# Two third-stage matmuls of a transform chunk placed side by side, each with its own accumulator bank

## The reference

```python
X = np.fft.rfft(x, axis=1)
Y = X * (filt_r + 1j * filt_i)[None]
x = np.fft.irfft(Y, n=3008, axis=1).reshape(6016, 256)
rms = np.sqrt(np.mean(x * x, axis=-1, keepdims=True) + 1e-06)
xn = x / rms * rms_g
g, val = xn @ w_gate, xn @ w_val                   # 256 x 1536 each
x = (g / (1 + np.exp(-g)) * val) @ w_out           # 1536 x 256
r = np.maximum(x @ w_in2, 0.0)                     # 256 x 2048
out = (s * (r * r) + b) @ w_out2                   # 2048 x 256
```

## Time and profile before

| | |
|---|---|
| median of 3 runs | 1290.36 us (1289.22 to 1291.53) |
| profiled execution | 1293.23 us, of which the recorded span is 1291.4 us |
| TensorE busy in the span | 1254.6 us (97%) |
| VectorE busy | 685.8 us (53%) |
| ScalarE busy | 564.6 us (44%) |
| GpSimd busy | 165.7 us (13%) |
| mean granted TensorE clock | 0.981 of full speed |

### The profile page before, as it was taken

One profiled execution on the slowest core, in us unless ns is written; L12 is line 12 of the kernel. 1 busy time (PEld: TensorE's weight loads), 2 busy tenths in 40 slices (PEclk: granted clock), 3 DMA queues, 4 the chain that ended last, 5 costly groups with the idle time before them and its releaser, 6 DMA issues.

```text
span 1291.4 us, 20490 instructions
## 1 busy us (share of the span) xinstructions
PE 1254.6 (97%) x7268; PEld 1220.7 (95%) x7268; DVE 685.8 (53%) x1161; ACT 564.6 (44%) x1122; POOL 165.7 (13%) x167
## 2 busy tenths in 40 slices
PE   8976899999999999999999999999999999999998
PEld 5644899999999999999999999999999999999998
DVE  3647345545445544445554366555655555555555
ACT  4625333433333334333344355455554555555544
POOL 5636111110111110111101030000000000000000
PEclk7978899999999999999999999999999999999999
DMA  8470600000000000000001000000000000000000
GB/s 234 136 202 11 177 14 13 13 13 2 10 12 12 12 12 0 12 12 12 0 14 51 1 1 13 13 13 13 12 12 12 12 12 12 12 12 12 4 9 24
DMA packets 20583, 37.91 MB, mean 29 GB/s; under 512 B 2240, under 2 KB 16192, under 8 KB 20288
## 3 DMA queue, kind: packets, MB, share of 16 engines
q1 hardware_dynamic: 20544, 37.40, 10.2%
HBM read 24.94 MB, written 12.45 MB: 29 GB/s over the span
## 4 chain that ended last, share of the span: by engine, by line
PE 89%; POOL 4%; issue 3%; DMA 2%; DVE 1%; ACT 1%; SPq 0%; POOLq 0%; ACTq 0%
PE bank L378 29%; PE bank L379 29%; PE bank L380 29%; POOL spec L877 2%; PE bank L365 2%; DMA by_j<-w_b 1%; POOL f L870 1%; DMA z_ring<-by_j 1%; POOL gate_lo L882 1%; PE bank L344 1%; DMA f<-filt 0%; PE bank L333 0%; PE bank L354 0%; PE bank L374 0%; PE bank L375 0%
## 5 line engine op out<-in xcount | busy, mean ns | idle before, releaser
L755 DVE TENSOR_TENSOR h<-bank,act 128x376 f32<-128x376 f32 x192 | 104.5, 545 | 307.4 <-PE bank L380 299.6
L793 DVE SCALAR_TENSOR_TENSOR h<-act,sc 128x376 f32<-128x376 f32 x256 | 159.5, 623 | 188.5 <-ACT act L621 184.5
L571 ACT ACTIVATE act<-bank 128x376 f32<-128x376 f32 x192 | 93.1, 485 | 374.6 <-PE bank L380 374.5
L621 ACT ACTIVATE act<-bank 128x376 f32<-128x376 f32 x256 | 124.1, 485 | 223.7 <-PE bank L380 223.6
L379 PE MATMUL bank<-h_lo,out_hi 128*128 128x376 f32 x512 | 171.4, 335 | 0.0
L380 PE MATMUL bank<-h_hi,out_lo 128*128 128x376 f32 x512 | 171.3, 335 | 0.0
L378 PE MATMUL bank<-xn_hi,in_hi 128*128 128x376 f32 x512 | 171.1, 334 | 0.2 <-issue 0.2
L378 PE MATMUL bank<-h_hi,out_hi 128*128 128x376 f32 x512 | 171.2, 334 | 0.0
L379 PE MATMUL bank<-xn_lo,in_hi 128*128 128x376 f32 x512 | 171.0, 334 | 0.0
L380 PE MATMUL bank<-xn_hi,in_lo 128*128 128x376 f32 x512 | 170.3, 333 | 0.0
L799 DVE SCALAR_TENSOR_TENSOR h_lo<-h,bi,h_hi 128x376 fp32r<-128x376 f32 x256 | 157.7, 616 | 0.2 <-ACT h_hi L630 0.2
(11 more groups left out here) (79 smaller groups left out, 2078.6 us busy)
## 6 DMA issues: line engine op xcount, KB each, us to landing
x_ring<-x SPq DMA_DIRECT2D x16, 384.0 KB, 5.6
by_j<-w_b SPq DMA_DIRECT2D x4, 1536.0 KB, 13.0
z_ring<-by_j SPq DMA_DIRECT2D x32, 192.0 KB, 2.9
out<-staged SPq DMA_DIRECT2D x32, 188.0 KB, 1.9
f<-filt SPq DMA_DIRECT2D x8, 384.0 KB, 7.8
in_raw<-w_in SPq DMA_DIRECT2D x1, 2048.0 KB, 7.9
out_raw<-w_out SPq DMA_DIRECT2D x1, 2048.0 KB, 8.3
gate_raw<-w_gate SPq DMA_DIRECT2D x1, 1536.0 KB, 13.0
```

Source lines behind the costliest of these rows:

```text
L571: nc.scalar.activation(act[:, c % 2], bank[2 * (c % 2)][:, 0:TILE], ACT.Silu).then_inc(silu_done, 1)
L621: nc.scalar.activation(act[:, c % 2], bank[c % 4][:, 0:TILE], ACT.Relu).then_inc(relu_done, 1)
L755: nc.vector.tensor_tensor(h[:, c % 2], bank[2 * (c % 2) + 1][:, 0:TILE], act[:, c % 2], ALU.mult).then_inc(hmul_done, 1)
L793: nc.vector.scalar_tensor_tensor(out=h[:, c % 2], in0=act[:, c % 2], scalar=sc2[:], in1=act[:, c % 2], op0=ALU.mult, op1=ALU.mult).then_in ...
```

## The change

Both third-stage matmuls of chunk q-1 are issued directly after `step2(q)`, and the first stage of chunk q+1 follows them. The half dp = 1 gets bank 7 in place of bank 6. ScalarE's two `w_out_copy` stand side by side in the same way, ahead of the two `u_out`. Since bank 7 is now shared, waits are added wherever the fourth stage, the sum of squares and the third stage follow each other in it, and `step4(1, 1, 1)` stands behind the last wait for `w_done` in place of ahead of it.

```diff
             def step3(q, dp):
                 pe.wait_ge(spec_done, 2 * q + dp + 1)
-                if q or dp:
-                    pe.wait_ge(w_done, 2 * q + dp)
-                nc.tensor.matmul(bank[6][:, 0:COLS], tabs[:, TB3:TB4], spec[:, q % 2, dp],
+                if q:
+                    pe.wait_ge(w_done, 2 * q + dp - 1)
+                if q in (11, 12, 15) and dp:
+                    pe.wait_ge(y_done, {11: 1, 12: 2, 15: 3}[q])
+                if q == 14 and dp:
+                    pe.wait_ge(var_done, 1)
+                nc.tensor.matmul(bank[6 + dp][:, 0:COLS], tabs[:, TB3:TB4], spec[:, q % 2, dp],
                                  start=True, stop=True).then_inc(s3_mm, 1)
...
                 if q == 12:
                     pe.wait_ge(consts_in, 64)
+                    pe.wait_ge(w_done, 2 * 11)
                     step4(0, 0, 0)
                 if q:
                     step3(q - 1, 0)
+                    step3(q - 1, 1)
                 if q + 1 < ALL:
                     step1(q + 1, 0)
                     step1(q + 1, 1)
-                if q:
-                    step3(q - 1, 1)
                 if q == 12:
+                    pe.wait_ge(w_done, 2 * 12)
                     step4(0, 0, 1)
                 if q == 14:
+                    pe.wait_ge(w_done, 2 * 14)
                     sums(0)
-            pe.wait_ge(var_done, 1)
+            pe.wait_ge(w_done, 2 * 15)
             step4(1, 1, 0)
             gate_val(0, 0, 0)
             step3(ALL - 1, 0)
             gate_val(0, 0, 1)
             step3(ALL - 1, 1)
+            pe.wait_ge(w_done, 2 * ALL)
             step4(1, 1, 1)
-            pe.wait_ge(w_done, 2 * ALL)
...
-                               bank[6][:, 0:COLS].rearrange("p (i g j) -> p j g i", i=PAIRS, g=HALVES)).then_inc(w_done, 1)
+                               bank[6 + dp][:, 0:COLS].rearrange("p (i g j) -> p j g i", i=PAIRS, g=HALVES)).then_inc(w_done, 1)
...
                 if q:
                     w_out_copy(q - 1, 0)
+                    w_out_copy(q - 1, 1)
                 if q + 1 < ALL:
                     u_out(q + 1, 0)
                     u_out(q + 1, 1)
-                if q:
-                    w_out_copy(q - 1, 1)
```

## The result

The changed kernel takes 1293.77 us (median of 16 runs, 1290.81 to 1299.17), the kernel before, run beside it, 1290.43 us (16 runs, 1288.98 to 1294.33). The ratio is 1.0028, 95% interval 1.0018 to 1.0039: slower by 3.3 us. A second measurement of the same pair gave 1.0026 (1.0012 to 1.0040). The forecast was 1292.0 us within 1288.6 to 1295.2, so the time is inside the range, but the likeliest case, no change by 0.2%, did not come. The loss is about twice the 1.66 us of the sum.

What follows compares the result with a forecast made beforehand. TensorE bounds the kernel after 126 us; before that, waits tied to stores and the normalised tile decide. Delays and gains up to `w_out_copy(15, 1)` sum to +1.66 on 1290.36, giving 1292.0 us, range 1288.6 to 1295.2.

Steps and rivals of the forecast that it cites:

- opening, up to turn 2: Before turn 2: one uncovered ScalarE copy starts that turn 0.75 us later, at 25.74.
- six turns from turn 2 to 8: Turns of 5.49 us with the copy uncovered: 32.94 us in place of 30.09; turn 8 starts 3.60 us later overall.
- release of the store within turn 8: The copy releasing batch 0's store comes 3.12 us into turn 8 in place of 4.87, 1.75 earlier.
- store to input of chunk 12: Chunk 12's input still lands 20.38 us behind the start of batch 0's store, SyncE's queue being the same.
- input to turn 12: After the input wait, at the lower clock, no third stage is left: 4.31 us in place of 4.99.
- turn 12: The added wait for `y_done` holds the second third-stage matmul: 8.80 us to turn 13 in place of 7.50.
- turn 15 to the gate product: With its own bank, `w_out_copy(14, 1)` comes 3.12 us into turn 15 in place of 3.98: 0.86 us won.
- I take zero: Nothing added for slow clock returns; upper bounds were 1.8 us after the second restart and 1.0 in turn 12.
- The clock stays up in the shortened wait: Rival, chance 0.10: clock holds through turn 11's halved input wait, taking 3.2 us off, to 1288.8 us.
- The clock falls inside the loop: Rival, chance 0.07: idle of about 0.6 us a turn drops the clock, 4.4 us per turn, 1305 us.
- Late clock: Rival, chance 0.18: clock returns late in turn 12 and after the second restart, adding 2.8 us, 1294.8 us.
- The copy not uncovered: Rival, chance 0.05: only 0.3 us of ScalarE's copy is uncovered, turns take 5.04 us, end 1288.9 us.

Runs made afterwards that it cites:

- the run from turn 8 on: Changed kernel's second bank and waits, old order in turns 1 to 7, new order in turns 8 to 15: 1290.29 us, ratio 0.9998 against the kernel before.
- the run with turn 8 and the clock held: Both banks, new order in turn 8 only, eight extra matmuls ahead of turn 11's first stage: 1286.49 us, ratio 0.9967 against the kernel before.
- the run that held it: Changed kernel plus six extra, never-read matmuls at the end of turn 11: 1289.86 us, ratio 0.9992 against the kernel before.
- `A`: Turn order of the kernel before (third, first, third stage), with the changed kernel's bank and waits; in every turn: 1291.23 us, ratio 1.0006 against before.
- `C`: Third-stage pair side by side behind the first stage, with the changed kernel's bank and waits; in every turn: 1290.89 us, ratio 0.9997 against before.
- turn 8 alone: Changed kernel's second bank and waits, new order in turn 8 only, old order in the other turns: 1288.31 us, ratio 0.9974 against the kernel before.

## Why the prediction was right or wrong

The chain that the sum followed was the right one, and each of its marks moved the way it was said to, as far as it can be told from the scatter. In numbers, with every trace of the same structure taken together (before twice; the changed order in four, of which the run from turn 8 on counts from that turn only):

| step | forecast | measured |
|---|---|---|
| opening, up to turn 2 | +0.75 | hidden in the scatter, see below |
| six turns from turn 2 to 8 | 32.94 us, +2.85 | 32.24 to 32.26 us; before 30.09 and 30.62: +1.9 |
| release of the store within turn 8 | -1.75 | -1.79 |
| store to input of chunk 12 | unchanged, 20.38 | 20.20 to 20.93, mean 20.55; before 20.16 and 20.38: +0.3 |
| input to turn 12 | 4.31, -0.68 | 4.29 to 4.30, -0.70 |
| turn 12 | 8.80, +1.30 | 10.48, 8.90, 10.42, 8.91, mean 9.68; before 7.50 and 6.94, mean 7.22: +2.46 |
| turns 13 and 14 | 10.98 | 10.98 |
| turn 15 to the gate product | -0.86 | -0.90 |
| gate product to second store | unchanged | 8.03 to 8.30, mean 8.13; before 7.76 and 7.51: +0.5 |
| second store to release by `z_ring` | unchanged | 26.51, 26.60, 27.26, 27.98, mean 27.09; before 26.67 and 26.63: +0.4 |

**The turn.** Uncovering the copy was right, and so was its size (2.49 us from first to second stage, 1.75 + 0.74). One term was too large: two third-stage matmuls side by side take 1.40 us and not 1.50. That is 0.1 a turn, 0.7 us over the six. The 0.75 us of the opening can't be read from turn 2's start. In traces in which the clock was back before turn 1, that turn took 5.37 to 5.83 us in the new order (four traces) and 4.84 to 4.99 in the old one (four), which bears the term out; a fifth, the run with turn 8 and the clock held, has 5.88 in the old order.

**Turn 12** is the term that was mis-sized. The step put it at 8.80 us by the wait for `y_done`, and that was right in two of four traces (8.90, 8.91). In the other two (10.48 and 10.42) the clock came back so late that it, and not the wait, set the turn. The upper bound I gave for this, 1.0 us, was too low (10.48 is 1.7 above 8.80), since it counted one third-stage matmul at the lower clock: in fact both and part of the first stage ran at it. And "I take zero" was the wrong choice, as the mean is 0.9 above 8.80. That the clock carries this term is shown by the run that held it: of its 3.8 us, 1.7 lie ahead of turn 12 and 1.0 to 2.6 in it.

Why the clock returns later is likely in the order after the wait. The old order has first stage, third stage, second stage, with TensorE busy throughout; the new one has first stage, a gap of 0.57 us, second stage. In the four traces with the gap the clock came back 7.7 to 12.5 us behind the restart. In the seven without it (before twice, the runs with `A` or `C` in turns 11 and 12 and no extra matmuls) it came back after 4.5 to 7.0. The two groups don't meet, but no run changed the gap alone, so that it is the gap is not shown.

**The clock stays up in the shortened wait** did not happen: the wait was 4.6 to 5.4 us in all traces of the changed order and the clock was down at its end in each. **The clock falls inside the loop** did not happen either; with 0.57 us idle in every turn it stood at 1.00 from 24 to 81 us of the first trace. The case that the Trainium skill describes on its page "TensorE: Matmul & The Clock Gate", section "A second HAM failure mode: psum-queue depth-cycling", in which short idle times between groups of matmuls make the clock go back and forth, is not this loop. Something like it shows in a place that I didn't name: in the ending, where waits of 0.57 and 1.10 us come close together, the clock fell at 133 us. It fell there in five of the ten traces with this ending and stayed at 1.00 in the other five, which have the same two waits, so the waits alone don't decide it. That fall lies ahead of the wait for `z_ring`. **Late clock**, given 0.18, is what half of the traces show, in turn 12 alone; the restart at the first gate product, for which it had 7.0 us, took 4.0 to 4.5 us in the four traces of the changed order and 2.9 and 3.4 before. The measured 1293.8 lies between the forecast's own case (1292.0) and this rival (1294.8). **The copy not uncovered** fell with the first trace.

**What was luck, and what stays open.** The forecast was too high by about 1.0 us for turns 2 to 8, of which 0.3 because these turns were short in the first trace of before, and it left out 1.2 us in turn 12 and another 1.2 in three stretches that it took as unchanged: store to input, gate product to second store, second store to `z_ring`. That the errors partly cancel is luck. With the measured terms, and 0.75 for the opening, the sum is 0.75 + 1.9 - 1.8 + 0.3 - 0.7 + 2.5 + 0.05 - 0.9 + 0.5 + 0.4 = 3.0 us, where the medians say 3.0 and 3.3 (2.3 to 5.0 and 1.5 to 5.2 us in the intervals). So close a match is luck too, as the means come from two and four traces that scatter by 0.6 to 1.6 us in turn 12 alone. The stretch up to the second store goes with the point at which the clock returns behind the first gate product: 7.51 and 7.76 us where it took 2.9 and 3.4 us, 8.03 to 8.30 where it took 4.0 to 4.5, and 8.76 with turn 8 alone, where it took 5.5. That the stretch from the second store to `z_ring` was longer in both traces of the changed kernel (27.26 and 27.98) and not in the two related runs (26.51 and 26.60) has no cause that the runs show.

## What to carry to other kernels

Before moving a matmul, look at what it hides: here a 0.75 us matmul ran while ScalarE made the copy that the next stage waits for. An ordinary turn took the same time whether one matmul or both stood there (4.76 us), and 0.6 us more when none did. Look next at what is released by the moved work and how long the queue behind it is: a store that starts 1.8 us sooner was worth more than the 0.6 us that a turn in the new order costs, so the new order paid in the single turn that releases the store and in no other that was tried. And cost a stretch behind a long wait at the lower clock, with the order of work as it stands there: behind the same kind of wait the clock was down for 7.0 us at most in the orders without a gap and for 12.5 at most in the order with one.

## What the runs showed of the hardware

The opening scatters more than the whole change: turn 2 started between 21.4 and 28.4 us over the traces. In the two traces of each kernel the clock fell at some point between 9.1 and 11.7 us and came back at some point between 15.1 and 24.0. The second trace of before shows an early return:

```profile
14.00:15.00 1.00, 1.00 (x6) 0.50 1.00 199
15.00:16.00 1.00, 0.83 (x7) 0.93 1.10 283
```

Turn 1 takes 4.99 us there and 7.31 us in the first trace of before. The spans of single traces can therefore not be compared (1291.4 and 1287.2 us for the kernel before, 1296.0 and 1291.7 for the changed one); they have to be compared stretch by stretch.

The read-back into `z_ring` was issued 17.1 to 17.5 us behind the start of the store in every trace but the first of before, where it was 79.90 - 60.46 = 19.4 us. The input of chunk 12, queued behind the same store, landed 20.1 to 20.9 us behind it in all of them. Why the one moved and the other did not is not known.
